# A three-stage fp32 block on one core: the last stage goes feature tile by feature tile, with six output tiles accumulating at once, and half of x is turned inside the MLP

## The chip, the core and the metric

One NeuronCore of a Trainium2 chip runs the whole program. The metric is device time in microseconds (us) of one execution, lower is better. TensorE is the matmul engine, VectorE and ScalarE the elementwise engines that can read PSUM, GpSimd the elementwise engine beside them (POOL in the rows), and SyncE issues most DMAs.

## The reference, cut to what matters

Masked attention over 2 batches, 8 heads, 768 tokens gives x (2 x 768 x 512). A Fourier mix, a normalisation and an MLP with 2048 hidden features follow, and then the last stage, which the change is about:

```python
def _moe2_ref(x, w_in, conv_w, w_out):        # x: 2 x 768 x 512, w_in: 512 x 1024, w_out: 1024 x 512
    h = np.maximum(x @ w_in, 0.0)
    hp = np.concatenate([zeros, h, zeros], axis=1)      # one token of padding at each end
    for k in range(3):
        conv_out += conv_w[k][None, None, :] * hp[:, k:k + S, :]
    gate = 1.0 / (1.0 + np.exp(-conv_out))
    return (h * gate @ w_out).astype(np.float32)
```

## The kernel before

Every fp32 product is made of three matmuls on operands split into a high and a low part (high x high, high x low, low x high); ScalarE writes a high part, and another engine the low part by subtraction. Each engine runs a program written out by hand, in order, and the engines meet only at semaphores: `wait_ge(sem, k)` holds an engine, and all that stands behind it, until the semaphore reaches k.

**The MLP.** Three blocks of 512 tokens. For each of 16 hidden tiles f, `up(f)` makes 12 matmuls into PSUM bank f % 2, ScalarE writes `hid_h`, VectorE `hid_l`, and `down(f - 1)` makes 12 matmuls into banks 4 to 7, so that all four token tiles of the block accumulate at once, three matmuls for each in turn. After the last `down`, VectorE adds four tiles to x (line 943).

**The last stage.** Its work comes in 16 rounds n, one for each batch b = n // 8 and tile f of 128 of the 1024 features. First x has to be turned (features on partitions): `turn_xt(b, m)` is three TensorE transposes (line 1261) into one bank, `store_xt` writes `xt_h` on ScalarE (L634) and `xt_l` on VectorE (L980); eight m per batch. Round n then runs:
- TensorE `widen(n)` (L1306): 24 matmuls of 384 columns, 12 for each half of the tokens, into banks 2 (n % 2) and the next.
- ScalarE `rectify(n)` (L642): one Relu per half into `act_s[n % 2]`; it counts `relu_done`.
- GpSimd (L476): `gate` = middle tap x `act_s`, once both halves are there.
- VectorE `convolve(n)` (L990): the two outer taps, two instructions one after the other.
- ScalarE Sigmoid on `gate` (L647), VectorE `apply_gate` (L996) multiplies by `act_s`, ScalarE writes the high part `g_h` (L649), and VectorE `gated_low` (L1001) or, in odd rounds below 8, GpSimd (L360) the low part `g_l`.

`g_h` and `g_l` hold all eight feature tiles of a batch. TensorE `narrow(r)` (L1320) then makes one output tile of 128 tokens from them: 24 matmuls of 512 columns into bank 6 + r % 2, for all eight f in a row. The 12 output tiles stand at the end of the stage: TensorE runs `widen(0)` to `widen(9)` with batch 1's turns behind the first six, then narrow(0) behind widen(10) and so on in turn, and the last seven `narrow` in a row. ScalarE copies each tile out (L655) and SyncE stores it.

Batch 0's x is turned at the end of the MLP: four m between the last `up` and the last `down`, four after it. GpSimd also makes the low part of `w_out`, `out_l` (L485), one tile a round in the first eight.

## Time and profile before

| | |
|---|---|
| time, median of 3 runs | 789.22 us (788.41 to 789.59) |
| the profiled execution: its time | 788.7 us |
| the profiled execution: its span | 786.9 us |
| TensorE busy | 738.2 us (94%) |
| VectorE, ScalarE, GpSimd busy | 418.3, 328.9, 251.2 us |
| the chain that ended last, by engine | TensorE 73%, VectorE 11%, ScalarE 8% |

The span is what the trace covers; the time is 1.8 us longer. An engine's busy time is a mean over stages with different limits; which wait counts has to be read from the chain that ended last and from the engines' rows in time order. A matmul's shown duration overlaps the next one's: the pace of a row of matmuls is the distance between their starts.

### The profile page before, as it was taken

What the parts mean: (1) busy time and instruction counts of PE and PEld (TensorE: products, weight loads), DVE (VectorE), ACT (ScalarE), POOL (GpSimd) and SP (SyncE); (2) the same over time, 40 slices, a digit from 0 to 9 for tenths busy, and PEclk for the clock granted to TensorE, in tenths of its full rate; (3) what the DMA queues carried; (4) which work ended last, traced back from release to release, by engine and by line L of the source; (5) the groups of instructions that cost most, each with busy time, mean ns of one, the idle gap of its engine ahead of it and who ended that gap; (6) DMA issues with size and microseconds to landing.
All of it is one profiled execution on the core that took longest, in us unless ns stands there. A gap on an engine that the chain in (4) does not pass through costs nothing.

```text
span 786.9 us, 11657 instructions
## 1 busy us (share of the span) xinstructions
PE 738.2 (94%) x4073; PEld 651.2 (83%) x4073; DVE 418.3 (53%) x787; ACT 328.9 (42%) x678; POOL 251.2 (32%) x244
## 2 busy tenths in 40 slices
PE   2899999999999997998999999999999988899998
PEld 1788888888888887997888888888888878898886
DVE  4688788887888888576421141113111158885320
ACT  2677777778777775221111111111101036443311
POOL 5555455556655504002840000000014034641000
PEclk9999999999999999999999999999999999999999
DMA  3223322223343102001310000001013042000011
GB/s 102 70 68 74 92 68 63 63 66 103 109 134 99 43 1 74 35 1 55 108 52 1 0 1 1 1 0 55 1 33 127 1 133 55 28 14 28 27 41 53
DMA packets 20450, 40.93 MB, mean 52 GB/s; under 512 B 2753, under 2 KB 7105, under 8 KB 19905
## 3 DMA queue, kind: packets, MB, share of 16 engines
q1 hardware_dynamic: 17968, 31.62, 14.3%
q0 software_dynamic: 2448, 8.87, 3.4%
q8 instruction: 21, 0.34, 0.2%
q14 instruction: 13, 0.10, 0.0%
HBM read 31.04 MB, written 3.15 MB: 43 GB/s over the span
## 4 chain that ended last, share of the span: by engine, by line
PE 73%; DVE 11%; ACT 8%; issue 6%; POOL 1%; DMA 0%; DVEq 0%; ACTq 0%; SPq 0%; POOLq 0%
PE ps L1162 23%; PE ps L1241 17%; PE ps L1320 9%; PE ps L1306 5%; PE ps L1083 4%; PE ps L1069 4%; PE ps L1057 3%; PE ps L1030 3%; ACT prob L512 2%; PE ps L1058 2%; ACT k L502 2%; DVE row_min L706 2%; ACT pt_h L524 1%; PE ps L1093 1%; ACT q L501 1%
## 5 line engine op out<-in xcount | busy, mean ns | idle before, releaser
L924 DVE SCALAR_TENSOR_TENSOR hid_l<-ps,hid_h 128x512 fp32r<-128x512 f32 x48 | 33.2, 691 | 203.0 <-ACT hid_h L612 203.0
L713 DVE TENSOR_TENSOR pt_l<-ps,pt_h 128x384 fp32r<-128x384 f32 x192 | 102.5, 551 | 47.5 <-ACT pt_h L524 47.2
L612 ACT ACTIVATE hid_h<-ps 128x512 fp32r<-128x512 f32 x48 | 28.7, 598 | 227.0 <-PE ps L1162 227.0
L524 ACT ACTIVATE pt_h<-ps 128x384 fp32r<-128x384 f32 x192 | 84.0, 489 | 48.8 <-PE ps L1069 48.2
L706 DVE TENSOR_REDUCE row_min<-ps 128x1 f32<-128x768 f32 x96 | 90.3, 940 | 6.5 <-PE ps L1058 6.5
L512 ACT ACTIVATE prob<-ps,row_min 128x768 f32<-128x768 f32 x96 | 86.8, 905 | 1.9 <-DVE row_min L706 1.5
L1069 PE MATMUL ps<-cst,prob 128*128 128x128 f32 x576 | 83.4, 282 | 2.9 <-ACT prob L512 2.8
L1057 PE MATMUL ps<-k,q 80*128 80x384 f32 x192 | 74.9, 390 | 3.4 <-ACT k L502 1.5
L1162 PE MATMUL ps<-un_h,w_h 128*128 128x512 f32 x192 | 75.7, 394 | 1.4 <-DVE un_l L918 1.4
L1241 PE MATMUL ps<-w_h,hid_h 128*128 128x512 f32 x192 | 76.0, 396 | 0.0
L1162 PE MATMUL ps<-un_l,w_h 128*128 128x512 f32 x192 | 75.6, 394 | 0.0
L1241 PE MATMUL ps<-w_h,hid_l 128*128 128x512 f32 x192 | 75.5, 393 | 0.0
L1162 PE MATMUL ps<-un_h,w_l 128*128 128x512 f32 x192 | 75.3, 392 | 0.0
L1241 PE MATMUL ps<-w_l,hid_h 128*128 128x512 f32 x192 | 74.7, 389 | 0.0
L1069 PEld LDWEIGHTS ps<-cst,prob 128*128 128x128 f32 x576 | 63.9, 144 | 11.6 <-ACT prob L512 4.3
L1058 PE MATMUL ps<-k,q 128*128 128x384 f32 x192 | 66.7, 348 | 0.0
L1083 PE MATMUL ps<-pt_h,v_n 128*128 128x384 f32 x192 | 64.9, 338 | 0.8 <-DVE x L770 0.6
L1083 PE MATMUL ps<-pt_l,v_n 128*128 128x384 f32 x192 | 64.9, 338 | 0.0
L454 POOL DMA_DIRECT2D in_h<-in_moe_w_in x4 | 2.2, 560 | 183.1 <-PE ps L1162 183.1
L990 DVE SCALAR_TENSOR_TENSOR gate<-act_s,taps,gate 128x768 f32<-128x768 f32 x32 | 43.0, 1343 | 9.4 <-POOL gate L476 8.8
L1306 PE MATMUL ps<-xt_h,in_h 128*128 128x384 f32 x128 | 43.8, 342 | 4.3 <-DVE xt_l L980 4.3
L1162 PEld LDWEIGHTS ps<-un_h,w_h 128*128 128x128 f32 x192 | 36.4, 190 | 9.5 <-DVE un_l L918 1.7
(138 smaller groups left out, 1570.8 us busy)
## 6 DMA issues: line engine op xcount, KB each, us to landing
stage<-in_moe_w_ch SPq DMA_DIRECT2D x16, 256.0 KB, 3.3
w_raw<-in_moe_w_ch SPq DMA_DIRECT2D x16, 256.0 KB, 2.6
raw_qk<-in_q SPq DMA_DIRECT2D x16, 192.0 KB, 3.2
raw_qk<-in_k SPq DMA_DIRECT2D x16, 192.0 KB, 3.4
raw_v<-in_v SPq DMA_DIRECT2D x16, 192.0 KB, 2.5
q<-q SPq DMA_DIRECT2D x16, 192.0 KB, 2.6
k<-k SPq DMA_DIRECT2D x16, 192.0 KB, 2.6
out<-out_s SPq DMA_DIRECT2D x12, 256.0 KB, 2.0
```

Source lines behind the costliest of these rows:

```text
L512: nc.scalar.activation(prob[t % 2][:, :, :].rearrange("p (h j) c -> p h (j c)", h=2), ps[:, 2 * (t % 2):2 * (t % 2) + 2, 0:HALF], ACT.Exp, ...
L524: nc.scalar.activation(pt_h[a][:, R * hf:R * hf + R, (t % R) * P:(t % R + 1) * P], ps[:, 4 + hf, 0:HALF].rearrange("p (j c) -> p j c", j=R ...
L706: nc.vector.tensor_reduce(row_min[:, col:col + 1], ps[:, 2 * (t % 2):2 * (t % 2) + 2, 0:HALF], axis=AX.XY, op=ALU.min).then_inc(min_ready, 1)
L713: nc.vector.tensor_tensor(pt_l[a][part], ps[:, 4 + hf, 0:HALF].rearrange("p (j c) -> p j c", j=R), as_f32(pt_h[a][part]), ALU.subtract).th ...
L1057: nc.tensor.matmul(bank, q2[s][0:D + C, cols], k2[s][0:D + C, keys], start=True, stop=False)
L1058: last = nc.tensor.matmul(bank, q1[s][:, cols], k1[s][:, keys], start=False, stop=True)
L1069: last = nc.tensor.transpose(ps[:, 4 + hf, j * P:(j + 1) * P], prob[t % 2][:, R * hf + j, :], ident)
L1083: last = nc.tensor.matmul(ps[:, 6, 0:HALF], v_n[s][:, j, :, :], src[:, j, :], start=j == 0 and src is pt_h[a], stop=j == NT - 1 and src is ...
L1162: last = nc.tensor.matmul(bank, st, mv, start=m == 0 and not open_already, stop=m == len(terms) - 1)
L1241: last = nc.tensor.matmul(ps[:, 4 + j, :], st[f % 2][:, toks], mv[:, f, :], start=f == 0 and n == 0, stop=f == FT - 1 and n == 2)
L1306: last = nc.tensor.matmul(bank, st[:, kt, cols], mv[:, kt, toks], start=kt == 0 and m == 0, stop=kt == KT - 1 and m == 2)
L1320: last = nc.tensor.matmul(ps[:, 6 + n % 2, :], st[:, f, toks], mv[:, f, :], start=f == 0 and m == 0, stop=f == FT2 - 1 and m == 2)
```

## The change

`narrow(n, tiles)` now belongs to round n, like `widen(n)`: it adds feature tile n's part to all six output tiles of the batch, three matmuls for each, into banks 2 to 7 (18 matmuls a round). It runs two rounds behind `widen` (`ROW_LAG`): TensorE's round n is widen(n), then narrow(n - 2). `widen` keeps banks 0 and 1 alone, one for each half, and waits for the `rectify` of the round before. `g_h` and `g_l` shrink to `g_ring`, four rounds deep; all low parts of it are VectorE's. Batch 1's turns use banks 0 and 1 too: two in each of rounds 2 to 5, behind the first three matmuls of `narrow`, and each waits for the Relu that empties its bank. ScalarE's round is now Sigmoid of n - 1, Relu of the first half, `gated_high(n - 1)`, Relu of the second half. VectorE does `apply_gate(n - 1)`, `gated_low(n - 1)`, the turned x, and `convolve(n)` last. The six output tiles of a batch end together, in round 9 and behind the last `widen`.

Of batch 0's x, the first four m are now turned behind up(2), up(4), up(6) and up(8) of the MLP's last block, the last four between its last `up` and its last `down`. The order of the two loops in TensorE's program, and all that it calls, is in the diff.

```diff
+XT_AT = (2, 4, 6, 8)
+XT_ROUNDS = range(ROW_LAG, ROW_LAG + KT)
+G_RING = 4
...
+        xt_0b = sb(late, "xt_0b", [2, KT // 2, S + 2], F32R)
+        g_ring = sb(late, "g_ring", [G_RING, 2, S], F32R)
...
-            return (2, 3, 0, 1, 4, 5, 6, 7)[m] if b == 0 else 4 + m % 2
-
-
-        XT_BEHIND = [(0, 1), (2, 3), (4,), (5,), (6,), (7,), (), ()]
+            return m % 2 if b or m >= 6 else 2 + m % 2
+
+
+        def xt_behind(n):
+
+            return (2 * (n - ROW_LAG), 2 * (n - ROW_LAG) + 1) if n in XT_ROUNDS else ()
+
+        def narrow_over(n):
+
+            if n % FT2 == FT2 - 1:
+                return row_ready, NT * (n // FT2 + 1)
+            return narrowed, n + 1 - n // FT2
...
             for n in range(B * FT2):
                 pool.wait_ge(relu_done, 2 * n + 2)
                 if n >= 2:
-                    pool.wait_ge(*low_done(n - 2))
+                    pool.wait_ge(g_low, n - 1)
                 nc.gpsimd.tensor_scalar(gate[n % 2][:, :], act_s[n % 2][:, 1:S + 1],
                                         taps[:, 1, n % FT2:n % FT2 + 1], 1.0, ALU.mult,
                                         ALU.mult).then_inc(tap_done, 1)
-                if n >= 1 and low_by_pool(n - 1):
-                    pool.wait_ge(g_high, n)
-                    low(g_l[0][:, n - 1, :], gate[(n - 1) % 2][:, :],
-                        as_f32(g_h[0][:, n - 1, :])).then_inc(g_low_pool, 1)
...
                 for f in range(FT):
                     store_hidden(blk, f)
+                    if not more and f in XT_AT:
+                        store_xt(0, XT_AT.index(f))
                     if first and f == 3:
                         act.wait_ge(var_done, 2)
...
-
-            def rectify(n):
-                for half in range(2):
-                    act.wait_ge(act_ready, 2 * n + half + 1)
-                    if n >= 2 and half == 0:
-                        act.wait_ge(gated, n - 1)
-                    nc.scalar.activation(act_s[n % 2][:, 1 + half * HALF:1 + (half + 1) * HALF],
-                                         ps[:, 2 * (n % 2) + half, 0:HALF], ACT.Relu).then_inc(relu_done, 1)
-
-            def gate_high(n):
+            def rectify(n, half):
+                act.wait_ge(act_ready, 2 * n + half + 1)
+                if n >= 2 and half == 0:
+                    act.wait_ge(gated, n - 1)
+                nc.scalar.activation(act_s[n % 2][:, 1 + half * HALF:1 + (half + 1) * HALF],
+                                     ps[:, half, 0:HALF], ACT.Relu).then_inc(relu_done, 1)
+
+            def open_gate(n):
                 act.wait_ge(conv_step, 2 * n + 2)
                 nc.scalar.activation(gate[n % 2][:, :], gate[n % 2][:, :], ACT.Sigmoid).then_inc(gate_done, 1)
+
+            def gated_high(n):
                 act.wait_ge(gated, n + 1)
-                nc.scalar.activation(g_h[n // FT2][:, n % FT2, :], gate[n % 2][:, :], ACT.Copy).then_inc(g_high, 1)
+                if n >= G_RING:
+                    act.wait_ge(*narrow_over(n - G_RING))
+                nc.scalar.activation(g_ring[:, n % G_RING, 0, :], gate[n % 2][:, :], ACT.Copy).then_inc(g_high, 1)
 
             def store_row(n):
                 act.wait_ge(row_ready, n + 1)
-                if n >= 2:
-                    act.wait_ge(out_written[n % 2], 16 * (n // 2))
-                nc.scalar.activation(out_s[:, n % 2, :], ps[:, 6 + n % 2, :], ACT.Copy).then_inc(row_stored, 1)
-
-            act.wait_ge(mlp_ready, B * NT)
-            for m in range(8):
+                if n >= NT:
+                    act.wait_ge(out_written[n % NT], 16)
+                nc.scalar.activation(out_s[:, n % NT, :], ps[:, 2 + n % NT, :], ACT.Copy).then_inc(row_stored, 1)
+
+            for m in range(4, 8):
                 store_xt(0, m)
             act.wait_ge(in_low, KT)
             for n in range(B * FT2):
-                rectify(n)
-                if n >= 1:
-                    gate_high(n - 1)
-                if n < FT2:
-                    for m in XT_BEHIND[n]:
-                        store_xt(1, m)
-                elif n >= FT2 + ROW_LAG:
-                    store_row(n - FT2 - ROW_LAG)
-            gate_high(B * FT2 - 1)
-            for n in range(FT2 - ROW_LAG, B * NT):
-                store_row(n)
+                if n >= 2:
+                    open_gate(n - 1)
+                rectify(n, 0)
+                if n >= 2:
+                    gated_high(n - 1)
+                rectify(n, 1)
+                for m in xt_behind(n):
+                    store_xt(1, m)
+                if n == 1:
+                    open_gate(0)
+                    gated_high(0)
+                if n == FT2 + ROW_LAG - 1:
+                    for m in range(NT):
+                        store_row(m)
+            open_gate(B * FT2 - 1)
+            gated_high(B * FT2 - 1)
+            for m in range(NT, 2 * NT):
+                store_row(m)
 
...
                     nc.vector.scalar_tensor_tensor(hid_l[f % 2][:, :], ps[:, f % 2, :], 0.0,
                                                    as_f32(hid_h[f % 2][:, :]), ALU.max,
                                                    ALU.subtract).then_inc(hid_low, 1)
+                    if not more and f in XT_AT:
+                        store_xt(0, XT_AT.index(f))
                     if first and f < 2:
...
             def gated_low(n):
                 dve.wait_ge(g_high, n + 1)
-                nc.vector.tensor_tensor(g_l[n // FT2][:, n % FT2, :], gate[n % 2][:, :],
-                                        as_f32(g_h[n // FT2][:, n % FT2, :]), ALU.subtract).then_inc(g_low, 1)
-
-            for m in range(8):
+                nc.vector.tensor_tensor(g_ring[:, n % G_RING, 1, :], gate[n % 2][:, :],
+                                        as_f32(g_ring[:, n % G_RING, 0, :]), ALU.subtract).then_inc(g_low, 1)
+
+            for m in range(4, 8):
                 store_xt(0, m)
             for n in range(B * FT2):
                 if n >= 1:
                     apply_gate(n - 1)
+                    gated_low(n - 1)
+                for m in xt_behind(n):
+                    store_xt(1, m)
                 convolve(n)
-                if n >= 1 and not low_by_pool(n - 1):
-                    gated_low(n - 1)
-                if n < FT2:
-                    for m in XT_BEHIND[n]:
-                        store_xt(1, m)
...
-            def turn_xt(b, m):
+            def turn_xt(b, m, after=0):
 
                 kt, a = m // 2, m % 2
                 if b:
                     pe.wait_ge(mlp_added, B * NT)
-                    pe.wait_ge(xt_low, 8 * b + m - 1)
+                    pe.wait_ge(relu_done, after)
                 elif m < 2:
                     pe.wait_ge(mlp_added, NT)
-                elif m < 4:
-                    pe.wait_ge(hid_low, FT * NBLK - 3 + m)
+                elif m < 6:
+                    pe.wait_ge(xt_low, m - 1)
                 else:
-                    pe.wait_ge(mlp_added, (NBLK - 1) * TBT + m - 3)
+                    pe.wait_ge(hid_low, FT * NBLK - 7 + m)
                 for r in range(R):
                     last = nc.tensor.transpose(ps[:, xt_bank(b, m), r * P:(r + 1) * P],
                                                x[:, b, R * a + r, kt * P:(kt + 1) * P], ident)
...
                 for f in range(1, FT):
                     up(blk, f)
+                    if not more and f in XT_AT:
+                        turn_xt(0, XT_AT.index(f))
                     if f == FT - 1 and more:
...
                 else:
-                    for m in range(4):
+                    for m in range(4, 8):
                         turn_xt(0, m)
                 down(blk, FT - 1)
...
             def widen(n):
                 b, f = n // FT2, n % FT2
-                if n >= 2:
-                    pe.wait_ge(relu_done, 2 * n - 2)
-                if n == FT2:
-                    pe.wait_ge(xt_low, 8 * b + 8)
-                if n == 0:
-                    pe.wait_ge(xt_low, 4)
                 for half in range(2):
+                    if n:
+                        pe.wait_ge(relu_done, 2 * n - 1 + half)
+                    if n - 1 in XT_ROUNDS:
+                        pe.wait_ge(xt_low, 8 + xt_behind(n - 1)[half] + 1)
                     toks, cols = slice(half * HALF, (half + 1) * HALF), slice(f * P, (f + 1) * P)
-                    bank = ps[:, 2 * (n % 2) + half, 0:HALF]
                     for kt in range(KT):
                         if n == 0:
-                            pe.wait_ge(xt_low, 2 * kt + half + 1)
+                            pe.wait_ge(xt_low, 8)
                             pe.wait_ge(in_low, kt + 1)
-                        for m, (st, mv) in enumerate(((in_h, xt_h[b]), (in_h, xt_l[b]), (in_l, xt_h[b]))):
-                            last = nc.tensor.matmul(bank, st[:, kt, cols], mv[:, kt, toks],
+                        hi, lo = xt_of(b, 0, kt), xt_of(b, 1, kt)
+                        for m, (st, mv) in enumerate(((in_h, hi), (in_h, lo), (in_l, hi))):
+                            last = nc.tensor.matmul(ps[:, half, 0:HALF], st[:, kt, cols], mv[:, toks],
                                                     start=kt == 0 and m == 0, stop=kt == KT - 1 and m == 2)
                     last.then_inc(act_ready, 1)
 
-            def narrow(n):
-                b, toks = n // NT, slice(n % NT * P, (n % NT + 1) * P)
-                if n >= 2:
-                    pe.wait_ge(row_stored, n - 1)
-                for f in range(FT2):
-                    if n % NT == 0:
-                        pe.wait_ge(*low_done(FT2 * b + f))
-                    if n == 0:
-                        pe.wait_ge(outw_low, f + 1)
-                    for m, (st, mv) in enumerate(((g_h[b], out_h), (g_h[b], out_l), (g_l[b], out_h))):
-                        last = nc.tensor.matmul(ps[:, 6 + n % 2, :], st[:, f, toks], mv[:, f, :],
+            def narrow(n, tiles):
+                b, f = n // FT2, n % FT2
+                hi, lo = g_ring[:, n % G_RING, 0, :], g_ring[:, n % G_RING, 1, :]
+                for t in tiles:
+                    toks = slice(t * P, (t + 1) * P)
+                    if t == 0:
+                        pe.wait_ge(g_low, n + 1)
+                        if n < FT2:
+                            pe.wait_ge(outw_low, f + 1)
+                        if n == 0:
+                            pe.wait_ge(mlp_added, B * NT)
+                    if b and f == 0:
+                        pe.wait_ge(row_stored, t + 1)
+                    for m, (st, mv) in enumerate(((hi, out_h), (hi, out_l), (lo, out_h))):
+                        last = nc.tensor.matmul(ps[:, 2 + t, :], st[:, toks], mv[:, f, :],
                                                 start=f == 0 and m == 0, stop=f == FT2 - 1 and m == 2)
-                last.then_inc(row_ready, 1)
-
-            for m in range(4, 8):
-                turn_xt(0, m)
+                    if f == FT2 - 1:
+                        last.then_inc(row_ready, 1)
+                    elif t == NT - 1:
+                        last.then_inc(narrowed, 1)
+
             for n in range(B * FT2):
                 widen(n)
-                if n < FT2:
-                    for m in XT_BEHIND[n]:
-                        turn_xt(1, m)
-                elif n >= FT2 + ROW_LAG:
-                    narrow(n - FT2 - ROW_LAG)
-            for n in range(FT2 - ROW_LAG, B * NT):
-                narrow(n)
+                if n >= ROW_LAG:
+                    narrow(n - ROW_LAG, range(0, 1))
+                    for half, m in enumerate(xt_behind(n)):
+                        turn_xt(1, m, after=2 * n + half + 1)
+                    narrow(n - ROW_LAG, range(1, NT))
+            for n in range(B * FT2 - ROW_LAG, B * FT2):
+                narrow(n, range(NT))
```

The rows below are what the engines run, in order, with what each row waits for; x12 is twelve of the same. TensorE in the first rounds, before: behind the last row of widen(2) comes turn_xt(1, 4), which waits only for the turned x before it (`xt_low`), and then widen(3).

```order
L1306 MATMUL ps<-xt_h,in_l 128x384
L1261 MATMUL ps<-cst,x 128x128 [waits xt_low,mlp_added]
L1261 MATMUL ps<-cst,x 128x128 x2
L1306 MATMUL ps<-xt_h,in_h 128x384 [waits relu_done]
L1306 MATMUL ps<-xt_l,in_h 128x384
```

TensorE behind widen(2) in the kernel after: L1337 is `narrow(0)`, L1274 is turn_xt(1, 0) and turn_xt(1, 1).

```order
L1337 MATMUL ps<-out_h,g_ring 128x512 [waits mlp_added,outw_low,g_low]
L1337 MATMUL ps<-out_l,g_ring 128x512
L1337 MATMUL ps<-out_h,g_ring 128x512
L1274 MATMUL ps<-cst,x 128x128 [waits relu_done,mlp_added]
L1274 MATMUL ps<-cst,x 128x128 x2
L1274 MATMUL ps<-cst,x 128x128 [waits relu_done,mlp_added]
L1274 MATMUL ps<-cst,x 128x128 x2
L1337 MATMUL ps<-out_h,g_ring 128x512
```

The rest of narrow(0), 15 matmuls, and widen(3) stand behind two waits for `relu_done`, and narrow(0) itself behind a wait for `g_low`.

ScalarE in the first rounds, before: `rectify(1)` (both halves), Sigmoid and high part of round 0, turned x, and then `rectify(2)`, both halves ahead of round 1's Sigmoid.

```order
L642 ACTIVATE act_s<-ps 128x384 [waits act_ready] x2
L647 ACT_TABLE_LOAD
L647 ACTIVATE gate<-gate 128x768 [waits conv_step]
L649 ACTIVATE g_h<-gate 128x768 [waits gated]
L634 ACTIVATE xt_h<-ps 128x3x128 [waits xt_turned] x2
L634 ACTIVATE xt_h<-ps 128x1
L642 ACTIVATE act_s<-ps 128x384 [waits gated,act_ready]
L642 ACTIVATE act_s<-ps 128x384 [waits act_ready]
L647 ACTIVATE gate<-gate 128x768 [waits conv_step]
```

ScalarE after, from the Relus of rounds 0 and 1 (L645) on; L650 is Sigmoid, L656 the high part, L619 the turned x.

```order
L645 ACTIVATE act_s<-ps 128x384 [waits act_ready] x3
L650 ACT_TABLE_LOAD
L650 ACTIVATE gate<-gate 128x768 [waits conv_step]
L656 ACTIVATE g_ring<-gate 128x768 [waits gated]
L650 ACTIVATE gate<-gate 128x768 [waits conv_step]
L645 ACTIVATE act_s<-ps 128x384 [waits gated,act_ready]
L656 ACTIVATE g_ring<-gate 128x768 [waits gated]
L645 ACTIVATE act_s<-ps 128x384 [waits act_ready]
L619 ACTIVATE xt<-ps 128x3x128 [waits xt_turned] x2
```

The first Relu of round 2 (second L645 row) now stands behind round 1's Sigmoid, and the second (third L645 row) behind round 1's high part.

## Rows read from the trace of the kernel before

**Rows 1.** The page, part 1: busy us, share of the span, instructions

```profile
PE 738.2 (94%) x4073; PEld 651.2 (83%) x4073; DVE 418.3 (53%) x787; ACT 328.9 (42%) x678; POOL 251.2 (32%) x244
```

**Rows 2.** Chain that ended last, 600 to 787 us: start us, us, what

```profile
630.46 2.77 PE ps L1241 x12
633.23 1.31 PE ps L1261 x12
634.53 2.77 PE ps L1241 x12
...
637.32 0.72 ACT xt_h L634
...
638.07 2.57 DVE xt_l L980 x6
...
640.69 4.75 PE ps L1306 x24
645.43 0.66 PE ps L1261 x6
...
700.95 4.25 PE ps L1306 x24
...
744.59 39.20 PE ps L1320 x168
...
783.82 0.60 ACT out_s L655
```

**Rows 3.** Busy us (x instructions) of each engine by stretch, PEclk, DMA share, GB/s

```profile
637.00:641.00 4.00, 1.93 (x16) 1.57 (x15) 3.94 (x9) 3.68 (x10) 0.00 (x0) 1.00 0.90 306
650.00:660.00 10.00, 7.98 (x47) 7.21 (x46) 8.35 (x14) 7.20 (x12) 3.18 (x4) 1.00 0.16 45
...
680.00:690.00 10.00, 7.73 (x44) 7.62 (x44) 8.24 (x9) 4.18 (x7) 6.45 (x5) 1.00 0.09 25
```

**Rows 4.** ScalarE in time order: start us, us, instruction, idle before and its releaser

```profile
650.33 0.49 ACT L642 ACTIVATE act_s<-ps 128x384 f32<-128x384 f32 x1 [1.60 <-PE ps L1306]
650.84 1.28 ACT L647 ACT_TABLE_LOAD   x1
652.14 0.85 ACT L647 ACTIVATE gate<-gate 128x768 f32<-128x768 f32 x1
654.01 0.85 ACT L649 ACTIVATE g_h<-gate 128x768 fp32r<-128x768 f32 x1 [1.03 <-DVE gate L996]
```

**Rows 5.** VectorE in time order, columns as in rows 4

```profile
635.26 2.75 DVE L943 TENSOR_TENSOR x<-x,ps 128x512 f32<-128x512 f32 x4 [3.44 <-PE ps L1241]
...
653.02 0.96 DVE L996 TENSOR_TENSOR gate<-gate,act_s 128x768 f32<-128x768 f32 x1 [1.58 <-ACT gate L647]
...
658.88 3.70 DVE L990 SCALAR_TENSOR_TENSOR gate<-act_s,taps,gate 128x768 f32<-128x768 f32 x2
...
680.66 0.95 DVE L1001 TENSOR_TENSOR g_l<-gate,g_h 128x768 fp32r<-128x768 f32 x1
...
710.51 2.07 DVE L990 SCALAR_TENSOR_TENSOR gate<-act_s,taps,gate 128x768 f32<-128x768 f32 x2 [0.81 <-POOL gate L476]
```

**Rows 6.** TensorE ahead of the MLP's first matmul, columns as in rows 4

```profile
362.28 1.04 PE L1210 MATMUL ps<-cst,stage 128*128 128x128 f32 x8
364.29 1.25 PE L1210 MATMUL ps<-cst,stage 128*128 128x128 f32 x8 [0.98 <-DVE un_l L918]
366.96 0.79 PE L1162 MATMUL ps<-un_h,w_h 128*128 128x512 f32 x1 [1.41 <-DVE un_l L918]
```

**Rows 7.** The same stretch by windows, columns as in rows 3

```profile
366.00:368.00 2.00, 1.04 (x3) 0.86 (x4) 2.00 (x6) 0.18 (x1) 1.92 (x3) 0.75 0.02 3
368.00:370.00 2.00, 2.00 (x6) 1.63 (x5) 2.00 (x7) 0.00 (x0) 0.94 (x1) 0.50 0.60 137
370.00:372.00 2.00, 2.00 (x9) 1.60 (x9) 0.87 (x3) 0.39 (x1) 0.43 (x1) 0.90 0.38 134
```

**Rows 8.** DMA issues, 700 to 787 us: count, KB each, median us to landing

```profile
out<-out_s SPq DMA_DIRECT2D x12, 256.0 KB, 2.0
```

More of the change, by code:

```diff
@@ L145, in build @@
         late = ExitStack()
-        g_h, g_l, xt_h, xt_l = [None] * B, [None] * B, [None] * B, [None] * B
-        g_l[1] = sb(late, "g_l1", [FT2, S], F32R)
+        sb(late, "x_of_0", [NT, DM])
+        out_s = sb(late, "out_s", [NT, DM])
         in_h = sb(late, "in_h", [KT, F2], F32R)
@@ L226, in build @@
         conv_step, gate_done, gated = sem("conv_step"), sem("gate_done"), sem("gated")
-        g_high, g_low, g_low_pool = sem("g_high"), sem("g_low"), sem("g_low_pool")
+        g_high, g_low, narrowed = sem("g_high"), sem("g_low"), sem("narrowed")
         row_ready, row_stored = sem("row_ready"), sem("row_stored")
-        out_written = [sem(f"out_written{j}") for j in range(2)]
+        out_written = [sem(f"out_written{j}") for j in range(NT)]
         block = main.enter_context(nc.Block())
@@ L346, in _ @@
                 sp.dma_start(out[n // NT, n % NT * P:(n % NT + 1) * P, :],
-                             out_s[:, n % 2, :]).then_inc(out_written[n % 2], 16)
-            for j in range(2):
-                sp.wait_ge(out_written[j], 16 * NT)
+                             out_s[:, n % NT, :]).then_inc(out_written[n % NT], 16)
+            for j in range(NT):
+                sp.wait_ge(out_written[j], 16 * B)
         @block.gpsimd
@@ L612, in store_hidden, with store_xt @@
                 nc.scalar.activation(hid_h[f % 2][:, :], ps[:, f % 2, :], ACT.Relu).then_inc(hid_high, 1)
+            def store_xt(b, m):
+                act.wait_ge(xt_turned, 8 * b + m + 1)
+                for dst, src in xt_parts(b, m, 0):
+                    last = nc.scalar.activation(dst, src, ACT.Copy)
+                last.then_inc(xt_high, 1)
             def mlp_block(blk, more, first=False):
@@ L919, in store_un, with store_xt @@
                                             ALU.subtract).then_inc(un_low, 1)
+            def store_xt(b, m):
+                dve.wait_ge(xt_high, 8 * b + m + 1)
+                for (dst, src), (high, _) in zip(xt_parts(b, m, 1), xt_parts(b, m, 0)):
+                    last = nc.vector.tensor_tensor(dst, src, as_f32(high), ALU.subtract)
+                last.then_inc(xt_low, 1)
             def mlp_block(blk, more, first=False):
@@ L974, in _ @@
             mlp_block(NBLK - 1, False)
-            def store_xt(b, m):
-                dve.wait_ge(xt_high, 8 * b + m + 1)
-                for (dst, src), (high, _) in zip(xt_parts(b, m, xt_l[b]), xt_parts(b, m, xt_h[b])):
-                    last = nc.vector.tensor_tensor(dst, src, as_f32(high), ALU.subtract)
-                last.then_inc(xt_low, 1)
             def convolve(n):
```

39 lines of the change are left out of this document (14 added, 25 removed).

## The prediction

> **What bounds the kernel now.** The page comes first: TensorE is busy for 94% of the span [rows 1], so the change can win only where TensorE waits, or by making its work shorter. The chain that ended last says where it waits in the last stage. It runs on TensorE to the end of the MLP's last `down` (634.53 + 2.77 = 637.30 us), passes through ScalarE and VectorE while batch 0's x is turned, and is back on TensorE at 640.69, when widen(0) starts [rows 2]. The time order of VectorE adds why: its four additions to x last until 638.01 [rows 5], and the turned x stands behind them. After that TensorE needs 16 widens at 4.25 us and 12 narrows at 39.20 / 7 = 5.60 us, 68.0 + 67.2 = 135.2 us, and eight turns at 0.66 / 2 = 0.33 us, 2.6 us; its last matmul ends with the last piece at 783.79 [rows 2]. From 640.69 that is 143.1 us, so 143.1 - 135.2 - 2.6 = 5.3 us are waits. The windows show them: 2.0 us between 650 and 660 and 2.3 us between 680 and 690 are not busy [rows 3]; there VectorE is busy 8.35 and 8.24 us of 10, so the elementwise engines pace those rounds. The clock is at its upper level, 2.4 GHz, in these windows. The last copy takes 0.60 us [rows 2], its store 2.0 us to land [rows 8].
>
> So 5.3 us is about all that a better order inside the stage can win, and 3.4 us (637.30 to 640.69) stands ahead of it.
>
> **The change, part by part.** I call the start of widen(0) zero, and walk the new order.
>
> *The MLP.* Four turns move ahead of the last `up`. Twelve transposes take 1.31 us [rows 2], so TensorE reaches the end of the last `down` 1.3 us later, 638.6. Their copies on ScalarE and VectorE are hidden: VectorE is idle 3.44 us ahead of its additions even at the end [rows 5]. The four turns that stood behind the last `down` ran 637.3 to 638.6 under VectorE's additions, so taking them away frees nothing. The additions now end at 638.0 + 1.3 = 639.3, and VectorE still has four low parts of x to make, 2.57 us as before [rows 2]; the other four are done. widen(0) used to start after four as well. It now starts at 641.9 instead of 640.69: **+1.2 us**. Range of this term: 0 if the turns cost nothing, 1.4.
>
> *TensorE's work from there.* 16 widens at 4.25 us, 68.0 us, unchanged. The narrows are the same 288 matmuls. Before, their pace is 39.20 / 168 = 0.2333 us. In the new order they walk over the output tiles three by three with the same moving operand, as `down` does, whose pace is 2.77 / 12 = 0.231 us [rows 2]. I take that one, being the same loop: 66.5 us instead of 67.2, **-0.7 us**, with 0 as the other end. Four pairs of turns at 0.66 us are 2.6 us.
>
> *The new waits.* widen(0), (1) and (2) run without narrows between them and end at 12.8. widen(1) ends at 8.5, its last matmul's result is out at about 8.8, and its second Relu ends at 9.3 (0.49) [rows 4]. From there the written order makes one chain of rounds 0 and 1, with no freedom in it: table load 1.28, Sigmoid 0.85 [rows 4], `apply_gate` 0.96 [rows 5], high part 0.85 [rows 4], `gated_low` 0.95 [rows 5]: 4.9 us, so that narrow(0) can start at 14.3, **1.5 us** late. Three matmuls, 0.7 us, to 15.0. Then turn_xt(1, 0) waits for the first Relu of round 2, which ScalarE may only do after round 1's Sigmoid, and that after `convolve(1)`, which stands behind `gated_low(0)` on VectorE: 14.2 + 2.07 [rows 5] + 0.85 + 0.49 [rows 4] = 17.6, **2.6 us** of waiting. The turn takes 0.33. turn_xt(1, 1) waits for the second Relu, now behind `apply_gate(1)` and the high part of round 1: 17.1 (Sigmoid's end) + 0.96 + 0.85 + 0.49 = 19.4: **1.5 us**. Together **5.6 us**. Behind these waits stand 15 matmuls of narrow(0) and widen(3), all that TensorE could do meanwhile. Later rounds take 4.25 + 4.2 = 8.4 us, 9.1 with turns. VectorE's part of one is at most 3.7 for a convolution that shares its time with GpSimd [rows 5], 0.96, 0.95 and 1.3 for two low parts of x (2.57 / 2): 6.9 us. GpSimd loses its low parts and keeps no one waiting. So no wait from round 3 on, and the last narrow finds its operands 7.6 us behind widen(15), with 8.4 us of narrows in between.
>
> *Sum.* 68.0 + 66.5 + 2.6 + 5.6 = 142.7, and 0.2 for the tail of the last matmul: 142.9 against 143.1. The stage itself breaks even: 5.3 us of old waits go and 5.6 of new ones come. With the start 1.2 us later, TensorE ends 1.0 us later.
>
> *The end.* Six output tiles now leave 0.7 us apart instead of 5.6. The busiest window moved 306 GB/s at a DMA share of 0.90 [rows 3], so 340 GB/s at full use, 0.77 us for 256 KB: the last tile is up to 5 x 0.07 = 0.35 us late; I take **0.2**. If they landed at 306 GB/s, 5.1 us for the six, it would be 1.0.
>
> Without anything else: +1.2 us.
>
> *The clock.* The new wait is long enough to ask whether the clock stays up. Between the last matmuls ahead of 362.3 and the MLP's first at 366.96 TensorE did 16 transposes and otherwise waited, 4.7 us [rows 6]; there the clock fell to 1.2 GHz, with means of 0.75, 0.50 and 0.90 in three windows, some 3.4 us in all at the lower level [rows 7]. At the end of the MLP it did 12 transposes in the 3.4 us without another matmul, and stayed at 1.00 [rows 2, 3]. In the new kernel there are 4.7 us (15.0 to 19.7) with six transposes, and 1.5 us of waiting with three matmuls shortly ahead. That is nearest to the first row. The price of 3.4 us at half clock is at most 1.7 us, if all of it meets matmuls; I take **1.3**, since it may begin before 19.7. The Trainium skill, "TensorE: Matmul & The Clock Gate", Part 4 (PE-mode transpose), says that transposes don't count as TensorE being busy. By it the six turns are no help, and the sum is +2.5 us; if they did help, it would be +1.2. Of the two stretches above, the first agrees with it, and the second doesn't settle it.
>
> **The rivals.**
> - *The clock stays up.* For it: the 3.4 us at the MLP's end, and three real matmuls in the middle. +1.2 us, **790.4**, a chance of 0.25.
> - *The first rounds are not paced as I walk them, and the waits nearly vanish* (the side of faster). If the second Relu of round 2 were there when TensorE is, the 5.6 us would go: 1.2 - 5.6 = -4.4, 784.8 us. It decides for faster once the chain from the second Relu of round 1 to that of round 2 (10.1 us) is under 7.3 us with the clock up. For it: the old order came through its first rounds with 2 us of waits. Against it: each link is a row at its shortest, and none can pass another. With what else I may have wrong in this direction: 0.15.
> - *The later rounds wait too.* ScalarE's Relu now stands between Sigmoid and high part, and rounds 3 to 5 must also bring two turned tiles each. The second turn of a round needs its Relu 1.0 us behind widen's end, and it is there 0.7 us behind it if ScalarE is free. Were VectorE's convolution 3.7 us [rows 5] in each of the three rounds, and the copies late by as much as that adds, 0.7 us a round would be lost, 2 us: 1.2 + 1.3 + 2 = +4.5, **793.7**, or the end comes 1 us late. 0.12.
>
> **How the numbers follow.** The profiled execution took 788.7 us, 1.8 over its span of 786.9, and stands 0.5 us under the median of the runs, 789.22. The forecast, start later, waits as many and one fall of the clock, is +2.5 us: 791.2 on its own time, 791.7 on the median. I give 791.4, chance 0.48; its own range is 790.3 to 792.6. The cases hold both signs; the range over all of them, 789.0 to 793.7, leaves out most of the faster case and the tail of the last. A measurement tells 0.2%, 1.6 us, from no change: slower is above 790.8. Forecast 0.42 of its 0.48, the last rival 0.12, clock up 0.05: slower 0.59. The rest of the two: same 0.26. Faster 0.15.
>
> **What the changed profile would show.** TensorE: the last `down` ending near 638.6, widen(0) at 641.9, narrow(0) some 14.3 us behind it, and three waits of 1.5, 2.6 and 1.5 us, for VectorE's low part and twice for ScalarE's Relu, then no wait to the end. PEclk at 0.5 for some 3 us around 660. Matmuls of narrow 0.231 us apart; the last store landing about 2.2 us after its copy. I am wrong if the waits around round 2 are under 3 us, if the clock is down for much longer, or if rounds 6 to 15 wait.

## The result, and the profile after

The changed kernel takes 791.89 us (median of five executions, 790.89 to 792.67) against 788.58 us for the kernel before in the same comparison; the ratio is 1.0038, 95% interval 1.0025 to 1.0051. It is slower, by 0.4%. The profiled execution took 791.89 us, with a span of 789.9 us. One further execution of it, at 929.23 us, and one at 1220.52 us in the run with the Relus first in round 2 were in a slow state, at mean clocks of 0.757 and 0.564, and are left out of every median here.

The chain that ended last, from the end of the MLP on (compare [rows 2]; columns start us, us, what):

```profile
632.47 1.31 PE ps L1274 x12
633.78 0.70 PE ps L1254 x3
...
634.50 0.69 DVE x L964
...
635.20 2.05 DVE x L964 x3
637.25 2.44 DVE xt_0b L937 x6
...
639.73 10.28 PE ps L1319 x48
...
650.03 0.49 ACT act_s L645
...
660.79 0.87 PE ps L1274 x3
661.67 5.08 PE ps L1337 x15
666.75 4.24 PE ps L1319 x24
...
765.69 4.20 PE ps L1337 x18
769.89 4.22 PE ps L1319 x24
774.12 12.66 PE ps L1337 x54
...
786.80 0.60 ACT out_s L662
```

The MLP ends in the same way as before, VectorE's additions and four low parts of x stand ahead of widen(0), and from 660.79 us to its last matmul the chain stays on TensorE. Between 650.03 and 660.79 it runs over ScalarE and VectorE, through the gates of rounds 0 and 1. From widen(0) to the last matmul it is 639.73 to 786.78 = 147.0 us, where it was 143.1. TensorE in time order, with the idle time ahead of a row and its releaser:

```profile
655.60 0.50 PE L1337 MATMUL ps<-out_h,g_ring 128*128 128x512 f32 x1 [1.38 <-DVE g_ring L1016]
...
658.92 0.88 PE L1274 MATMUL ps<-cst,x 128*128 128x128 f32 x3 [2.37 <-ACT act_s L645]
660.79 0.87 PE L1274 MATMUL ps<-cst,x 128*128 128x128 f32 x3 [0.99 <-ACT act_s L645]
```

The waits of 1.38, 2.37 and 0.99 us are the three that were forecast, for `gated_low(0)` and for the two Relus of round 2. The three transposes behind a wait last 0.88 us, where six in a row took 0.66 us at the upper clock [rows 2]. Part of it is the start behind a wait: three take 0.52 us there with the clock up, as the run with unused matmuls shows below. The rest is the clock (windows: us, busy of each engine, PEclk, DMA share, GB/s):

```profile
640.00:642.00 2.00, 2.00 (x11) 2.00 (x11) 0.00 (x0) 0.00 (x0) 0.00 (x0) 0.78 0.02 7
642.00:644.00 2.00, 2.00 (x8) 2.00 (x7) 0.00 (x0) 0.49 (x1) 0.00 (x0) 0.50 0.00 0
644.00:646.00 2.00, 2.00 (x12) 2.00 (x11) 0.00 (x0) 0.21 (x1) 0.00 (x0) 0.86 0.00 0
...
658.00:660.00 2.00, 0.88 (x3) 0.51 (x3) 0.96 (x1) 1.35 (x3) 0.00 (x0) 0.55 0.00 0
660.00:662.00 2.00, 1.21 (x5) 1.14 (x6) 1.67 (x2) 1.54 (x4) 1.25 (x1) 0.50 0.00 0
662.00:664.00 2.00, 2.00 (x6) 1.54 (x5) 1.54 (x3) 0.43 (x2) 1.29 (x2) 0.50 0.04 8
664.00:666.00 2.00, 2.00 (x8) 1.59 (x7) 1.18 (x2) 0.75 (x1) 0.00 (x0) 0.74 0.51 131
```

By these means the clock stands at its lower level twice: for 3.4 us from 641.1 us, 1.4 us behind the start of widen(0), and for 6.8 us from 658.2 us, in the waits of round 2 and the matmuls behind them. The first was not forecast. It makes the first 48 matmuls of `widen` 10.28 us long instead of 8.75 (the rerun below). The second was, but with half its length, the 3.4 us of [rows 7].

### The profile page after: what moved, and what is told of

Its sections match the earlier page's. It is cut to its first block, busy times and chain, and to the rows that moved or that the text cites. A ratio compares the mean times of both kernels' runs of the same rounds, so it can differ in the third digit from the quotient of the medians.

```text
span 789.9 us, 11673 instructions
## 1 busy us (share of the span) xinstructions
PE 741.1 (94%) x4073; PEld 653.7 (83%) x4073; DVE 415.9 (53%) x791; ACT 330.7 (42%) x678; POOL 236.8 (30%) x240
## 3 DMA queue, kind: packets, MB, share of 16 engines
q1 hardware_dynamic: 17968, 31.62, 14.3%
## 4 chain that ended last, share of the span: by engine, by line
PE 75%; DVE 10%; ACT 8%; issue 6%; DMA 0%; POOL 0%; DVEq 0%; ACTq 0%; SPq 0%; POOLq 0%
PE ps L1175 23%; PE ps L1254 17%; PE ps L1337 9%; PE ps L1319 8%; PE ps L1096 4%; PE ps L1082 4%; PE ps L1070 3%; PE ps L1043 3%; PE ps L1071 2%; ACT prob L514 2%; ACT k L504 2%; DVE row_min L719 2%; ACT pt_h L526 1%; PE ps L1106 1%; ACT q L503 1%
## 5 line engine op out<-in xcount | busy, mean ns | idle before, releaser
L1337 PE MATMUL ps<-out_h,g_ring 128*128 128x512 f32 x192 | 64.9, 404 | 1.4 <-DVE g_ring L1016 1.4
L482 POOL TENSOR_SCALAR gate<-act_s,taps 128x768 f32<-128x768 f32 x16 | 14.9, 930 | 116.2 <-ACT act_s L645 116.2
L1005 DVE SCALAR_TENSOR_TENSOR gate<-act_s,taps,gate 128x768 f32<-128x768 f32 x32 | 35.6, 1114 | 22.5 <-POOL gate L482 22.0
```

The costliest lines, as they stand in the source:

```text
L1337: last = nc.tensor.matmul(ps[:, 2 + t, :], st[:, toks], mv[:, f, :], start=f == 0 and m == 0, stop=f == FT2 - 1 and m == 2)
```

## The experiments

Each was timed beside the kernel before on its own chip. Ratios are to that, so they can be compared across jobs; medians only within one.

**The changed kernel again.** No edit.

> The changed kernel itself, unaltered, as the mark for the runs beside it. Both theories expect what was measured: 3 to 4 us over the kernel before. If the falls of the clock are a matter of where a stall meets a clock that runs by itself, its single times should lie in two or three groups about 1.5 us apart, lower with a higher mean clock.

Measured: 791.91 us against 788.83, ratio 1.0042 (1.0029 to 1.0055). In its profiled execution the clock fell once in the last stage, from 657.3 us, again for 6.8 us. The pieces of its chain that answer to those above:

```profile
634.41 1.31 PE ps L1274 x12
...
641.66 8.75 PE ps L1319 x48
...
661.20 0.88 PE ps L1274 x3
662.08 4.48 PE ps L1337 x15
666.56 4.24 PE ps L1319 x24
```

The start of widen(0) lies 7.25 us behind the start of the twelve transposes, in the kernel before 7.46 [rows 2]. All of it stands 1.2 us later in the program than before (634.41 against 633.23 us, each with two falls of the clock upstream), which fits the four turns in the MLP. From 641.66 to 786.58, the end of its last matmul, it is 144.9 us. Over this job and the comparison above, the two executions of the changed kernel with a mean clock of 0.996 took 790.89 and 791.02 us, the eight with 0.991 took 791.68 to 793.16: the groups are there, if less clean than expected.

**Relus first, in round 2 alone** (ScalarE).

```diff
+                if n == 2:
+                    rectify(n, 0)
+                    rectify(n, 1)
+                    open_gate(n - 1)
+                    gated_high(n - 1)
...
```

> In round 2 alone ScalarE does both Relus first, then the Sigmoid and the high part of round 1. Theory A (the two turns of round 2 wait for Relus that stand behind round 1's Sigmoid and high part, and the clock falls in that stretch): the waits of 2.4 and 1.0 us ahead of the turns go, the one of 1.4 us ahead of the first narrow stays, and the fall of the clock near 660 us goes with them, worth 1.3 to 1.6 us: 4 to 5 us faster than the changed kernel, 787 to 788. Rival B (the chain Sigmoid, gate, high part, low part of rounds 0 and 1 sets the pace of the first rounds, wherever the Relus stand): TensorE waits as long, one step later, for the low part of round 1, and the time stays within 1 us of the changed kernel.

Measured: 789.87 us, ratio 1.0015 (1.0006 to 1.0024), 2.0 us under the changed kernel in the same job. Neither theory had it. TensorE in time order:

```profile
655.73 0.50 PE L1343 MATMUL ps<-out_h,g_ring 128*128 128x512 f32 x1 [1.38 <-DVE g_ring L1022]
...
662.75 0.59 PE L1325 MATMUL ps<-xt_0a,in_h 128*128 128x384 f32 x2 [1.89 <-DVE xt L943]
```

The two waits ahead of the turns are gone, and a wait of 1.9 us stands ahead of widen(3), for the turned tiles, whose low parts VectorE may only write behind `gated_low(1)`. 3.4 us of waits went, 1.9 came back, and the clock still fell, from 663.6 us on, but for 3.4 us instead of 6.8.

**Batch 0's turns back** where the kernel before has them (TensorE; ScalarE and VectorE store all eight behind the MLP).

```diff
-                    if not more and f in XT_AT:
-                        turn_xt(0, XT_AT.index(f))
...
-                    for m in range(4, 8):
+                    for m in range(4):
                         turn_xt(0, m)
...
+            for m in range(4, 8):
+                turn_xt(0, m)
             for n in range(B * FT2):
                 widen(n)
```

> Batch 0's turns go back to where they were, four between the last up and the last down of the MLP and four behind the last down; the last stage stays as changed. Theory A (the four turns cost TensorE 1.3 us in the MLP and give nothing back, since VectorE still has four low parts of x to make behind its additions): widen(0) starts 1.3 us earlier and the time falls by 1.3 us, to some 790.7. Rival B (turning early takes work off VectorE's path): widen(0) starts later, or runs with waits between its matmuls, and the time rises by up to 2.5 us.

Measured: 790.33 us, ratio 1.0021 (1.0011 to 1.0030), 1.6 us under the changed kernel in the same job. Theory A's sign and, within what single times scatter (789.45 to 792.26), its size. In its profiled execution TensorE waits 1.9 us ahead of widen(0) instead of 3.2. The clock is low again for 6.8 us near round 2, but until 5.9 us behind the start of the second turn, in the rerun until 2.9, so that more of it meets matmuls: the 15 of narrow(0) behind the turns take 5.84 us, in the rerun 4.48.

**Unused matmuls in the waits** (TensorE).

```diff
+            def fill(bank, count):
+                for _ in range(count):
+                    nc.tensor.matmul(ps[:, bank, :], in_h[:, 0, 0:P], in_h[:, 0, 0:512], start=True, stop=True)
...
+            fill(4, 12)
             for n in range(B * FT2):
                 widen(n)
+                if n == 2:
+                    pe.wait_ge(mlp_added, B * NT)
+                    fill(7, 5)
...
+                        if n == 2:
+                            fill(7, (9, 3)[half])
                         turn_xt(1, m, after=2 * n + half + 1)
```

> The changed kernel with matmuls whose result nobody uses, put where TensorE waits: 12 ahead of widen(0), 5 ahead of the first narrow, 9 and 3 ahead of the two turns of round 2. They take 0.23 us each and fit into the waits of 3.2, 1.4, 2.4 and 1.0 us. Theory A (the waits also let the clock fall, at widen(0) and again near round 2, for some 3.4 us each): PEclk stays at 1.00 from 637 us on, the 48 matmuls of widen(0) to widen(1) take 8.5 us instead of 10.3, and the time is 2.5 to 3 us lower than the changed kernel's, 789 to 790. Rival B (the clock costs nothing, since the chain of the other engines sets these rounds): no gain, or a loss of some tenths of a us from matmuls that overrun their wait.

Measured: 790.53 us, ratio 1.0021 (1.0012 to 1.0029), 1.4 us under the changed kernel in the same job. TensorE around round 2, and the windows:

```profile
655.19 0.50 PE L1337 MATMUL ps<-out_h,g_ring 128*128 128x512 f32 x1 [0.22 <-DVE g_ring L1016]
...
658.52 0.52 PE L1274 MATMUL ps<-cst,x 128*128 128x128 f32 x3 [0.29 <-ACT act_s L645]
...
660.40 0.52 PE L1274 MATMUL ps<-cst,x 128*128 128x128 f32 x3 [0.65 <-ACT act_s L645]
```

```profile
641.00:650.00 9.00, 9.00 (x52) 9.00 (x53) 2.93 (x2) 1.85 (x4) 2.16 (x2) 1.00 0.08 14
...
656.00:662.00 6.00, 5.06 (x25) 3.69 (x24) 3.98 (x6) 3.77 (x7) 1.65 (x2) 1.00 0.00 0
662.00:668.00 6.00, 6.00 (x33) 5.54 (x32) 3.88 (x6) 2.07 (x3) 0.91 (x1) 1.00 0.17 44
```

The chain of the other engines is as long as before: the second turn starts 19.5 us behind widen(0) (640.86 to 660.40), as in the rerun (641.66 to 661.20). Only the idle time has shrunk to 0.2, 0.3 and 0.7 us, and the clock is at its upper level from 641 us on. From widen(0) to the last matmul this execution took 143.6 us against 144.9. So keeping the clock up in the last stage is worth 1.3 us in this pair of profiled executions, where the rerun has one fall of 6.8 us, and the medians differ by 1.4. That is not the 2.5 to 3 expected, which had counted a fall at widen(0) too; the rerun's profiled execution had none there, and how many of the others had one was not recorded.

**Batch 1's turns one round later**, in rounds 3 to 6.

```diff
-XT_ROUNDS = range(ROW_LAG, ROW_LAG + KT)
+XT_FIRST = 3
+XT_ROUNDS = range(XT_FIRST, XT_FIRST + KT)
...
```

> One number changed: batch 1's turns stand in rounds 3 to 6 instead of 2 to 5. Nothing of ScalarE's or VectorE's order around round 2 moves but the turned tiles. Theory A (round 2 waits because banks 0 and 1 are wanted for the turns there, while the other engines are still at the gates of rounds 0 and 1): TensorE waits only ahead of the first narrow, 1.4 us; the waits of 2.4 and 1.0 us go, and in most executions the fall of the clock near 660 us: 4 to 5 us under the changed kernel's 791.9, so 787 to 788. Rival B (the chain of the gates sets the pace, as the run with the Relus first half showed, where 1.9 us of waiting came back ahead of the next widen): the waits come back in round 3, and the time falls by 2 us or less.

Measured: 790.75 us, ratio 1.0025 (1.0016 to 1.0034): 1.3 us by the ratios, rival B. The waits moved with the turns:

```profile
669.01 0.52 PE L1275 MATMUL ps<-cst,x 128*128 128x128 f32 x3 [1.56 <-ACT act_s L646]
670.88 0.87 PE L1275 MATMUL ps<-cst,x 128*128 128x128 f32 x3 [1.35 <-ACT act_s L646]
```

ScalarE in time order shows what they wait for:

```profile
652.47 0.49 ACT L646 ACTIVATE act_s<-ps 128x384 f32<-128x384 f32 x1 [1.60 <-PE ps L1320]
...
661.87 0.85 ACT L657 ACTIVATE g_ring<-gate 128x768 fp32r<-128x768 f32 x1 [0.65 <-DVE gate L1012]
662.62 0.48 ACT L646 ACTIVATE act_s<-ps 128x384 f32<-128x384 f32 x1
667.64 0.84 ACT L651 ACTIVATE gate<-gate 128x768 f32<-128x768 f32 x1 [4.55 <-DVE gate L1006]
...
669.51 0.84 ACT L657 ACTIVATE g_ring<-gate 128x768 fp32r<-128x768 f32 x1 [0.65 <-DVE gate L1012]
670.26 0.47 ACT L646 ACTIVATE act_s<-ps 128x384 f32<-128x384 f32 x1
```

GpSimd and VectorE in the same stretch:

```profile
663.19 1.29 POOL L483 TENSOR_SCALAR gate<-act_s,taps 128x768 f32<-128x768 f32 x1 [7.94 <-ACT act_s L646]
664.51 3.09 DVE L1006 SCALAR_TENSOR_TENSOR gate<-act_s,taps,gate 128x768 f32<-128x768 f32 x2 [0.81 <-POOL gate L483]
```

The second Relu (L646) comes at 652.47, 662.62 and 670.26 us, in rounds 1, 2 and 3. Round 3's stands behind the high part of round 2 (L657), this behind gate and Sigmoid (L651, 667.64), this behind the convolution (L1006) and GpSimd's tap (L483), which could not begin before the second Relu of round 2 was there. It is a loop through ScalarE's written order, 7.6 us a round behind a first lap of 10.1 us, and TensorE arrives early at it with the first turns in round 2 and in round 3. My theory so far, that it was the place of the turns in round 2, falls. The single times lie in steps: 789.46 to 789.90 us at a mean clock of 0.995, 790.57 to 791.73 at 0.993, 793.10 at 0.991.

**The table load off the chain**, with the turns in rounds 3 to 6.

```diff
+            nc.scalar.activation(ln[:, 0:1, 8], ln[:, 0:1, 8], ACT.Sigmoid)
             act.wait_ge(in_low, KT)
...
```

> The turns in rounds 3 to 6, and a Sigmoid of one column, whose result nobody reads, on ScalarE ahead of the first Relu of the last stage, so that the table load of 1.28 us falls into ScalarE's wait for widen(0). Theory A (the first narrow waits for the chain table load, Sigmoid, gate, high part, low part): its wait goes from 1.4 to 0.1 us and the time falls by another 1.3 us. Rival B (ScalarE loads a table again at the real Sigmoid, or the chain is late elsewhere): no change against the run with the turns alone.

Measured: 790.13 us, ratio 1.0022 (1.0012 to 1.0032). The wait ahead of the first narrow went from 1.37 to 0.20 us, as expected, but the ratio moved by 0.0003 alone, which the intervals don't tell from nothing; the waits in round 3 are as long as before:

```profile
653.70 0.50 PE L1339 MATMUL ps<-out_h,g_ring 128*128 128x512 f32 x1 [0.20 <-DVE g_ring L1018]
...
664.67 0.52 PE L1276 MATMUL ps<-cst,x 128*128 128x128 f32 x3 [1.56 <-ACT act_s L646]
666.54 0.87 PE L1276 MATMUL ps<-cst,x 128*128 128x128 f32 x3 [1.35 <-ACT act_s L646]
```

**The same, and batch 0's turns back.**

> As the run before, and batch 0's turns back behind the MLP's last up and last down. By the 1.3 us that the turns cost in the MLP, 1.3 to 1.6 us faster again: some 785. If the early turns pay once the other waits are gone, it is slower instead.

Measured: 788.56 us, ratio 0.9996 (0.9986 to 1.0006), 1.6 us under the run before: the second time that the turns in the MLP cost that much. The 785 expected did not come. With this, the kernel is level with the one before. Its times again lie in two groups, 786.76 to 787.51 us at a mean clock of 0.995 and 788.41 to 789.31 at 0.993.

**The same with the turns in the MLP, and 12 unused matmuls ahead of widen(0).**

> As the run with late turns and early table, batch 0's turns in the MLP, and 12 unused matmuls in the wait of 3.2 us ahead of widen(0). If the clock falls at widen(0) in part of the executions, the median is up to 1 us lower than without them and the times lie closer together; if it falls there in few, there is no difference.

Measured: 790.61 us, ratio 1.0022 (1.0012 to 1.0032): nothing against the run without them (790.13 us), and about as much scatter (786.92 to 791.51 against 787.99 to 793.13). In the profiled execution the clock stays up at widen(0), but near round 3 it is low for 6.8 us, where the run without the unused matmuls had 3.4. How many executions fall at widen(0) stays open; the profiled ones are counted in the last section.

**Relus first in rounds 2 to 7, turns in rounds 4 to 7.** The edit of the second experiment with `if 2 <= n < 8`, and `XT_FIRST = 4`.

> ScalarE does both Relus first in rounds 2 to 7, and batch 1's turns stand in rounds 4 to 7. After the runs with late turns the theory is changed. Theory A2 (a loop through ScalarE's order: the second Relu of a round stands behind the high part of the round before, that behind the gate, the Sigmoid, the convolution and the tap, which wait for the second Relu of that round; it takes some 8 us a round from where round 1 left it, and any turn that wants a Relu's bank early waits for it, in round 2 or in round 3; with the Relus first the loop is cut, and by round 4 VectorE's turned tiles have found room): the waits of 2.4 and 1.0 us vanish and no others take their place, only 1.4 us ahead of the first narrow stay; 3.4 us and a fall of the clock less than the changed kernel, 787.0 to 788.0. Rival B2 (VectorE itself is short of time in the first rounds): waits of 2 to 4 us come back in rounds 2 to 5, and the time stays near 790.

Measured: 787.86 us against 787.81, ratio 1.0000 (0.9989 to 1.0010), 3.3 us under the changed kernel by the ratios. TensorE waits 1.4 us ahead of the first narrow and 0.7 us in all, in four pieces of 0.2, ahead of the widens that need turned tiles. The waits of 2.4 and 1.0 us are gone, and no long one took their place. Two things were changed at once here; the last run parts them.

**And the table load off the chain.**

> As the run before, with the table load taken off the chain. Theory A2: TensorE waits only 0.2 us after widen(0) starts; 1.2 us less than the run before. By rows of TensorE: 68.0 us of widens, 67.2 of narrows at the pace measured in the changed kernel, 2.6 of turns and 0.3, 138 us from widen(0) to the last matmul against 143.1 in the kernel before: about 786.5. B2: no gain over the run before.

Measured: 787.38 us, ratio 0.9995 (0.9984 to 1.0006): 0.5 us less than the run before, in the direction of the 1.2 expected and not told from nothing. In the profiled execution the wait ahead of the first narrow is down to 0.2 us; the stage takes 141.7 us (640.38 to 782.11) instead of the 138 expected, with a fall of the clock at widen(0).

**And batch 0's turns back.**

> As the run before, and batch 0's turns behind the MLP's last up and last down as in the kernel before. Another 1.3 us off: about 785, 3 to 4 us faster than the kernel before, the rounds by feature tile then being worth what the old order's waits cost.

Measured: 785.28 us against 787.81, ratio 0.9960 (0.9945 to 0.9974), as expected in the total; 2.1 us under the run before, the third time that the turns in the MLP cost more than 1.3 us.

**And batch 1's turns in rounds 3 to 6.**

> As the run before, but batch 1's turns in rounds 3 to 6. If it is the Relus alone that the turns waited for, no difference. If VectorE is still behind in round 3 (it has the low part of round 2, two turned tiles and a convolution there), widen(4) waits for the turned tiles some 0.5 to 1.5 us, and the time is that much higher.

Measured: 784.57 us, ratio 0.9957 (0.9941 to 0.9973). No difference beyond the scatter to rounds 4 to 7. This version and the one before it beat both kernels.

This run also isolates the loop. Its kernel differs from that of the run with late turns, early table and batch 0's turns back (788.56 us, ratio 0.9996) in the order of ScalarE's Relus in rounds 2 to 7 and in nothing else. There TensorE still waited ahead of the turns of round 3:

```profile
664.86 0.52 PE L1272 MATMUL ps<-cst,x 128*128 128x128 f32 x3 [1.57 <-ACT act_s L644]
666.73 0.52 PE L1272 MATMUL ps<-cst,x 128*128 128x128 f32 x3 [1.35 <-ACT act_s L644]
```

Behind these waits its clock was low for 3.4 us, and from widen(0) to the last matmul it took 143.4 us (640.47 to 783.86). With the Relus first both waits and the fall are gone, and it is 140.2 us: 3.1 us less by the traces and 3.1 by the ratios.

The chain that ended last, from widen(0) on, and whom TensorE waited for from 652 us on (us in total, times, longest):

```profile
639.07 4.76 PE ps L1321 x24
...
652.47 4.48 PE ps L1339 x18
...
666.24 4.47 PE ps L1321 x24
...
766.66 12.66 PE ps L1339 x54
...
779.34 0.60 ACT out_s L661
```

```profile
PE ps L1321 <- DVE xt L943: 0.7, 4, 0.2
PE ps L1339 <- DVE g_ring L1020: 0.2, 1, 0.2
```

From widen(0) at 639.07 to the end of the last matmul (766.66 + 12.66) it is 140.2 us, 2.9 less than in the kernel before; the clock is at its upper level in all of it. The rows of full pace come to 68.0 + 67.2 + 2.6 = 137.8 us. What is left is the 0.9 us of idle time, the restart behind each of these five waits (the first 18 narrows 4.48 instead of 4.20 us, each of the four widens 4.47 to 4.49 instead of 4.24, 1.2 us), and widen(0) at 4.76, 0.5 us; these come to 2.6 us for the 2.4 there are, since the other widens take 4.22 to 4.24 us and not 4.25.

## Why the prediction was right, point by point

The direction and the size held: +2.5 us forecast, +3.3 measured between the medians (+3.0 by the ratio), inside the range. The waits, which decide the direction, came as walked. That the size came so near is partly luck, since several terms were off both ways. By its steps:

- *TensorE sets the end, so waits decide.* Right. The chain is on TensorE from 660.79 us on, and nothing waits later than round 2. But not all of the 5.3 us counted as old waits was idle time: the trace of before shows some 4.2 us of it, and 0.5 us was widen(0) at 4.75 us [rows 2], which the new order keeps.
- *The four turns move into the MLP and make widen(0) 1.2 us later.* Right. The rerun shows 1.2 us at the transposes, 1.0 at widen(0) (641.66 against 640.69 us), and putting them back was worth 1.6, 1.6 and 2.1 us. What the step took for nothing is the place that the turns left: with no turns behind the last `down`, TensorE waits 3.2 us ahead of widen(0) without a matmul, where it waited 2.1, and only behind the longer wait did the clock fall there (last section).
- *The new waits, 1.5, 2.6 and 1.5 us.* Right in place, order and releaser; measured 1.38, 2.37 and 0.99, 4.7 us instead of 5.6, the third shorter mostly because the transposes ahead of it ran slowly. The chain was walked to 14.3, 17.6 and 19.4 us behind widen(0); in the rerun the three rows stand at 14.4 (656.01), 17.7 and 19.5 us.
- *No wait from round 3 on.* Right for the changed kernel. The reason given, VectorE's busy time per round, was not what limits: the experiments with late turns found a loop of 7.6 us through ScalarE's order, which is shorter than TensorE's own round of 8.4 to 9.1 us. In the changed kernel it stays hidden once TensorE has waited for it in round 2.
- *The narrows at the pace of `down`, -0.7 us.* Wrong. 54 matmuls take 12.66 us, 18 take 4.20: 0.233 to 0.234 us, the pace of before. The same loop form did not give the same pace; why `down` is quicker wasn't tried.
- *The end, +0.2 us.* From the last copy's start to the end of the span it is 789.9 - 786.80 = 3.1 us; before, 786.9 - 783.82 = 3.1 us. Six tiles 0.7 us apart cost nothing more than one.
- *The fall of the clock near round 2, +1.3 us.* Right that it falls, and in the rerun it costs 0.35 us in each turn and 4.48 - 3.50 = 1.0 us in the narrow behind them, 1.7 us. The term was mis-sized: the clock was low for 6.8 us, not for the 3.4 of [rows 7]. Its price depends on how much of that time meets matmuls: the 15 matmuls behind the turns lose 1.0 us in the rerun, where the clock is back 2.9 us behind the start of the second turn, 1.6 in the first profiled execution (4.2 us), and 2.3 with batch 0's turns back (5.9 us). What I missed is the other fall, at widen(0), 1.5 us in the executions that have it (10.28 against 8.75 us). The first profiled execution had both; its stage of 147.0 us is the rerun's 144.9, these 1.5, and 0.6 of the narrow (5.08 against 4.48).

The sum for the rerun: 68.0 + 67.2 + 2.6 + 4.7 of waits + 0.2 of tail + 1.7 for the clock = 144.4 us against 144.9 measured. The 0.5 us missing is about what the sum leaves out, slow starts: widen(0) and (1) take 8.75 us instead of 8.5, and each of the two turns behind a wait 0.2 us more than 0.33 with the clock up. The 0.7 us that the pace didn't give and the waits that were 0.9 shorter nearly cancelled, and the start and the end, 0.2 less each, made up for the clock's larger share. The rivals: the clock did not stay up in either profiled execution; the faster case did not happen, and the argument against it, that a chain of written order can't be passed, is what the experiments bore out, until that order was changed; waits in later rounds came only in kernels that put the first turns later or, ahead of widen(3), did the Relus first in round 2 alone.

## What to carry to other kernels

A stage that interleaves two products has a start, in which nothing covers the elementwise chain: walk it instruction by instruction from the last matmul that doesn't depend on it, and keep every release of a PSUM bank ahead of whatever ends a longer chain in the same engine's order. If a wait merely moves when its waiter is moved, it is a loop through some engine's order; look for the instruction that closes it, here a Relu behind the previous round's gate, and move that. Work moved off a wait that another engine would have caused anyway costs its full length where it lands.

## What the runs showed of the hardware

- The same program's clock fell once in the last stage in one profiled execution (the rerun) and twice in another. With the turns in rounds 3 to 6 the times lie in groups 1 to 2 us apart, lower with a higher mean clock; in other runs such groups overlap. A difference of 1 us between single executions says nothing here.
- Seven profiled executions, of kernels with batch 0's early turns and no unused matmuls, waited 3.2 us ahead of widen(0); in three of them (the changed kernel, the late turns, the early Relus with the early table) the clock fell 0.7 to 1.4 us behind its start. In the five whose last four turns stand behind the last `down`, the kernel before among them, the wait was 1.9 to 2.1 us and the clock did not fall there; nor did it in the two with unused matmuls in the wait.
- Unused matmuls in all four waits left the clock at its upper level through the stage in the profiled execution, and delayed nothing (the second turn still 19.5 us behind widen(0)). Those ahead of widen(0) alone changed the median by nothing that can be told.
- A table load took 1.28 us on the chain, and the Sigmoid behind it started within 0.02 us of its end [rows 4]. With a one-column Sigmoid ahead of the stage no load stood there, and the wait of 1.37 us fell to 0.20.
